# Decays and queries of a chunked decay attention read straight out of PSUM, one pair of score banks, a weight split moved to GpSimd

## The reference

```
for t in range(S):
    cur = einsum('bhd,bhe->bhde', u * k[t], v[t])
    y[t] = einsum('bhd,bhde->bhe', r[t], state + cur)
    state = w[t] * state + einsum('bhd,bhe->bhde', k[t], v[t])
x = moe(y)                                # 4 experts, causal softmax, top 2
out = x + relu(norm(x) @ w_ch1) @ w_ch2
```

## Time and profile before

| | us |
|---|---|
| median of 3 runs | 906.62 |
| lowest, highest | 905.15, 911.12 |
| span of the profiled execution, first to last instruction | 907.4 |
| busy in it: TensorE, VectorE, ScalarE, GpSimd | 843.7, 489.2, 362.3, 145.4 |
| mean granted clock of TensorE | 0.941 of full |

### The profile page before, as it was taken

One profiled execution on the slowest core, in us unless ns is written; L12 is line 12 of the kernel. 1 busy time (PEld: TensorE's weight loads), 2 busy tenths in 40 slices (PEclk: granted clock), 3 DMA queues, 4 the chain that ended last, 5 costly groups with the idle time before them and its releaser, 6 DMA issues.

```text
span 907.4 us, 16347 instructions
## 1 busy us (share of the span) xinstructions
PE 843.7 (93%) x5962; PEld 787.3 (87%) x5962; DVE 489.2 (54%) x1022; ACT 362.3 (40%) x714; POOL 145.4 (16%) x127
## 2 busy tenths in 40 slices
PE   3878877777999999999999999999999999999998
PEld 3777776677889889999988999998899999889998
DVE  4899999999753565222356522225562232556221
ACT  4666665756413454112344411234441123444111
POOL 4464656555400000000000000000000000000000
PEclk8587979978669999999999999999999999999999
DMA  5544645544330000000100000010000000000000
GB/s 152 149 96 104 162 104 108 171 116 91 71 122 1 1 1 1 18 18 22 52 1 1 1 18 18 20 54 1 1 1 19 18 10 10 1 1 2 18 18 18
DMA packets 94007, 40.69 MB, mean 45 GB/s; under 512 B 73712, under 2 KB 93296, under 8 KB 93936
## 3 DMA queue, kind: packets, MB, share of 16 engines
q1 hardware_dynamic: 93664, 38.55, 16.5%
q0 software_dynamic: 272, 1.18, 0.4%
HBM read 30.19 MB, written 9.54 MB: 44 GB/s over the span
## 4 chain that ended last, share of the span: by engine, by line
PE 75%; DVE 19%; issue 4%; ACT 1%; DMA 1%; DVEq 0%; POOL 0%; SPq 0%; ACTq 0%; POOLq 0%
PE sc_ps L1302 26%; PE tp L1420 17%; PE mx_ps L1342 8%; DVE grow L899 4%; DVE state L937 4%; PE tp L1330 4%; PE sc_ps L1437 3%; DVE suf L883 3%; PE tp L1302 3%; PE mx_ps L1302 3%; PE mx_ps L1437 2%; PE sc_ps L1319 2%; PE y_ps L1263 2%; DVE w_lo L957 1%; DVE at L915 1%
## 5 line engine op out<-in xcount | busy, mean ns | idle before, releaser
L858 ACT ACTIVATE hT_hi<-sc_ps 128x256 fp32r<-128x256 f32 x144 | 55.4, 385 | 203.0 <-PE sc_ps L1302 203.0
L1302 PE MATMUL sc_ps<-aT_hi,w_hi 128*128 128x256 f32 x432 | 123.5, 286 | 0.0
L1302 PE MATMUL sc_ps<-aT_hi,w_lo 128*128 128x256 f32 x432 | 122.3, 283 | 0.0
L1302 PE MATMUL sc_ps<-aT_lo,w_hi 128*128 128x256 f32 x432 | 122.2, 283 | 0.0
L1010 DVE TENSOR_REDUCE nmax<-sc_ps 128x1 f32<-128x768 f32 (+2 forms) x96 | 59.8, 623 | 87.6 <-PE sc_ps L1319 86.5
L684 POOL TENSOR_TENSOR rstd<-vare,power 128x1 f32<-128x1 f32 x24 | 13.2, 550 | 567.8 <-DVE vare L1058 567.8
L1181 DVE SCALAR_TENSOR_TENSOR hT_lo<-sc_ps,hT_hi 128x256 fp32r<-128x256 f32 x144 | 60.7, 424 | 72.8 <-ACT hT_hi L858 72.2
L1420 PE MATMUL tp<-w_hi,hT_hi 128*128 128x384 f32 x288 | 97.3, 338 | 0.0
L1420 PE MATMUL tp<-w_hi,hT_lo 128*128 128x384 f32 x288 | 96.8, 336 | 0.0
L1420 PE MATMUL tp<-w_lo,hT_hi 128*128 128x384 f32 x288 | 96.7, 336 | 0.0
L1263 PE MATMUL y_ps<-vc,at 128*128 128x64 f32 x384 | 71.5, 323 | 14.7 <-DVE state L928 8.9
(11 more groups left out here) (170 smaller groups left out, 1799.6 us busy)
## 6 DMA issues: line engine op xcount, KB each, us to landing
nat_w<-in_w SPq DMA_DIRECT2D x16, 288.0 KB, 3.3
nat_k<-in_k SPq DMA_DIRECT2D x16, 288.0 KB, 3.6
nat_r<-in_r SPq DMA_DIRECT2D x16, 288.0 KB, 3.9
vc<-in_v SPq DMA_DIRECT2D x32, 144.0 KB, 2.8
stage<-in_moe_w_ch SPq DMA_DIRECT2D x6, 768.0 KB, 5.6
x_scratch<-ystage SPq DMA_DIRECT2D x16, 288.0 KB, 3.0
out<-ost SPq DMA_DIRECT2D x24, 192.0 KB, 1.9
xs<-x_scratch SPq DMA_DIRECT2D x3, 1152.0 KB, 5.9
```

What stands on the lines that cost most here:

```text
L858: nc.scalar.activation(hT_hi[:, n % FT, :], sc_ps[:, n % 4 // 2, n % 2, 0:TF], ACT.Relu).then_inc(h_hi, 1)
L1302: last = pe.matmul(o, a, c, start=(i == 0), stop=(i == len(ops) - 1), skip_group_check=True)
```

## The change

- w is loaded with two neighbouring positions per partition and three blocks of 256 positions (runs of 384 bytes in DRAM in place of 1152), and its six transpositions write into a PSUM tile of its own, `w_ps`, with a step of two columns, so that w lies there in the order of time. The scans of `decays` and `growth` read w_ps; wT and its copy are gone. `decay_rows` transposes two units ahead, behind outputs(1) and ahead of key_values.
- r stays in PSUM in the order (c, p). `queries` moves from GpSimd to VectorE, multiplies it there by grow with a strided view of PSUM, and writes qhat; rT and its copy are gone. k is still copied by ScalarE, now with the stride on the side of the PSUM read.
- `a_ps` has one pair of banks instead of two, so `pairs` of one half waits for `masked` of the other.
- The low part of each w_ch2 piece is computed by GpSimd behind khat.
- `sums` moves behind `y_half` 1; semaphores are split accordingly.

```diff
-        wT = sb("wT", [P, S], on=p1)
-        rT = sb("rT", [P, S], on=p1)
+        w_ps = pb("w_ps", [P, 2 * 512], on=q1)
         tp1 = pb("tp1", [P, 2 * 512], on=q1)
-        a_ps = pb("a_ps", [P, G, 2, 512], on=q1)
+        a_ps = pb("a_ps", [P, 2, 512], on=q1)
...
+                sp.dma_start(nat_w[:, i % 2, :, :].rearrange("p h (j x) -> p h j x", j=PAIRS),
+                             of_unit(w, b, i).rearrange("b h (j p c) d -> p (b h) j (c d)", p=P, c=2)
+                             ).then_inc(rkw_in[i % 2], 16)
...
-            def queries(un, i):
-                pool.wait_ge(tp_out, prep_use(un, 2) + 1)
-                pool.wait_ge(grow_ok, un + 1)
-                pool.tensor_tensor(qhat[:, i % HP, :], rT[:, :], grow[:, :], ALU.mult).then_inc(qhat_ok, 1)
...
+            def low(piece, n):
+                staged, hi, lo, _ = piece
+                pool.wait_ge(stage_hi, n + 1)
+                pool.tensor_tensor(lo, staged, hi.bitcast(F32), ALU.subtract).then_inc(w2_split, 1)
...
-                    queries(un + 1, i + 1)
+                if not isinstance(un, int) and i >= 2:
+                    low(ffn_piece(b, 1, i - 2), b * (2 * CUTS) + (i - 2) * 2 + 1)
...
-                nc.scalar.activation(in_time((wT, kT, rT)[j][:, :]),
-                                     prep_bank(un, j).rearrange("x (c p) -> x c p", c=NR),
-                                     ACT.Copy).then_inc(tp_out, 1)
+                nc.scalar.activation(kT[:, :].rearrange("x (p c) -> x p c", c=NR),
+                                     tp1[:, 0:S].rearrange("x (c p) -> x p c", c=NR), ACT.Copy).then_inc(k_out, 1)
...
-                    done = dve.tensor_tensor_scan(backwards(suf, first, last - 1), backwards(wT, first + 1, last),
+                    done = dve.tensor_tensor_scan(backwards(suf, first, last - 1), backwards(w_ps, first + 1, last),
                                                   ones[:, 0:C - 1], 1.0, ALU.mult, ALU.mult)
...
-                    done = dve.tensor_tensor_scan(grow[:, first + 1:first + C], wT[:, first:first + C - 1],
+                    done = dve.tensor_tensor_scan(grow[:, first + 1:first + C], w_ps[:, first:first + C - 1],
                                                   ones[:, 0:C - 1], grow[:, first:first + 1], ALU.mult, ALU.mult)
...
+            def queries(un, i):
+                dve.wait_ge(r_full, un + 1)
+                dve.wait_ge(grow_ok, un + 1)
+                dve.tensor_tensor(qhat[:, i % HP, :].rearrange("x (p c) -> x p c", c=NR),
+                                  r_bank(un).rearrange("x (c p) -> x p c", c=NR),
+                                  grow[:, :].rearrange("x (p c) -> x p c", c=NR), ALU.mult).then_inc(qhat_ok, 1)
...
+            def decay_rows(un):
+                pe.wait_ge(pad_ok, un * PREP + 1)
+                if not isinstance(un, int) or un:
+                    pe.wait_ge(grow_ok, un)
+                for c in range(NR):
+                    first = c // 2 * (2 * P) + c % 2
+                    last = pe.transpose(w_ps[:, first:first + 2 * P - 1:2], channels(pad_w, c), ident[:, :])
+                last.then_inc(w_full, 1)
...
                 pe.wait_ge(khat_ok, un + 1)
-                pe.wait_ge(tp_out, khat_use(un))
+                pe.wait_ge(qhat_ok, un + 1)
...
-                if i >= 1:
-                    pe.wait_ge(at_ok, un * G + g - 1)
+                if i >= 1 or g:
+                    pe.wait_ge(at_ok, un * G + g)
```

More of the change, by code:

```diff
@@ L30, in build @@
     RUN = NR * D
+    PAIRS = S // (2 * P)
     PW = 2 * D
@@ L196, in build @@
         pad_ok = sem("pad_ok")
-        tp_full = sem("tp_full")
-        tp_out = sem("tp_out")
+        w_full = sem("w_full")
+        k_full = sem("k_full")
+        k_out = sem("k_out")
+        r_full = sem("r_full")
+        back_full = sem("back_full")
+        khn_ok = sem("khn_ok")
+        w2_split = sem("w2_split")
         suf_ok = sem("suf_ok")
@@ L314, in build, with r_bank @@
         PREP = 3
[L316 to L327, removed]
+        def r_bank(un):
+            if isinstance(un, int) and un == 0:
+                return a_ps[:, :, :].rearrange("p a n -> p (a n)")[:, 0:S]
             return tp1[:, 0:S]
@@ L972, in _ @@
             growth(0, 0)
-            dve.wait_ge(tp_out, prep_use(0, 1) + 1)
+            dve.wait_ge(k_out, 1)
             dve.tensor_tensor(khat[:, 0, :], kT[:, :], suf[:, :], ALU.mult).then_inc(khat_ok, 1)
-            dve.wait_ge(tp_out, prep_use(0, 2) + 1)
-            dve.wait_ge(grow_ok, 1)
-            dve.tensor_tensor(qhat[:, 0, :], rT[:, :], grow[:, :], ALU.mult).then_inc(qhat_ok, 1)
+            queries(0, 0)
             sums(0)
@@ L996, in turn @@
                     growth(un + 1, i + 1)
-                if exists(un + 1):
                     masked(un, i, 1)
-                    sums(un + 1)
+                    queries(un + 1, i + 1)
                 if i >= 1:
                     y_half(un - 1, i - 1, 1)
+                if exists(un + 1):
+                    sums(un + 1)
                 if not isinstance(un, int) and i >= 2:
-                    for n in range(2):
-                        low(ffn_piece(b, n, i - 2), b * (2 * CUTS) + (i - 2) * 2 + n)
+                    low(ffn_piece(b, 0, i - 2), b * (2 * CUTS) + (i - 2) * 2)
             def maxima(b, n):
@@ L1192, in _ @@
             y_half(NU - 1, HP - 1, 0)
-            low(expert_piece(0), IN_LOOP)
+            low(expert_piece(0), 2 * IN_LOOP)
             y_half(NU - 1, HP - 1, 1)
@@ L1196, in _ @@
             for n in (1, 2):
-                low(expert_piece(n), IN_LOOP + n)
+                low(expert_piece(n), 2 * IN_LOOP + n)
             sequences(dve, walk)
@@ new lines, in key_rows, with query_rows @@
+            def key_rows(un):
+                pe.wait_ge(pad_ok, un * PREP + 2)
+                if not isinstance(un, int) or un:
+                    pe.wait_ge(khn_ok, un)
+                for c in range(NR):
+                    last = pe.transpose(tp1[:, c * P:(c + 1) * P], channels(pad_k, c), ident[:, :])
+                last.then_inc(k_full, 1)
+            def query_rows(un):
+                pe.wait_ge(pad_ok, un * PREP + 3)
+                if not isinstance(un, int) or un:
+                    pe.wait_ge(k_out, un + 1)
+                for c in range(NR):
+                    last = pe.transpose(r_bank(un)[:, c * P:(c + 1) * P], channels(pad_r, c), ident[:, :])
+                last.then_inc(r_full, 1)
@@ L1232, in pairs @@
                         o = (c - g * GC) * C
-                        last = pe.matmul(a_ps[:, g, hh, o:o + C], khat[rows, i % 2, cs], qhat[rows, i % HP, cs],
+                        last = pe.matmul(a_ps[:, hh, o:o + C], khat[rows, i % 2, cs], qhat[rows, i % HP, cs],
                                          start=True, stop=True)
@@ L1267, in _ @@
             pe.wait_ge(const_ok, 4)
-            for j in range(PREP):
-                to_channels(0, j)
+            decay_rows(0)
+            key_rows(0)
+            query_rows(0)
+            decay_rows(1)
             def turn(un, b, i):
@@ L1288, in turn @@
                 if exists(un + 1):
-                    to_channels(un + 1, 1)
+                    key_rows(un + 1)
                 pairs(un, i, 1)
                 if exists(un + 1):
-                    to_channels(un + 1, 2)
+                    query_rows(un + 1)
                 if i >= 1:
                     outputs(un - 1, i - 1, 1)
+                if exists(un + 2):
+                    decay_rows(un + 2)
                 key_values(un, b, i)
```

89 lines of the change are left out of this document (42 added, 47 removed).

## The result

| | us |
|---|---|
| before, median of 4 runs beside it | 908.87 (905.15 to 912.07) |
| changed, median of 4 runs | 885.97 (885.20 to 887.25) |
| ratio | 0.9749, 95% interval 0.9718 to 0.978 |
| profiled execution: span before, after | 907.4, 883.7 |

A forecast was written before the change was run, and what follows sets the result against it. VectorE was taken to set the pace in the first stage. Turns -17.3, start -3.4 and TensorE's clock +5 sum to -15.7 us, from the median of 906.62 to 890.9, say 891; range 883 to 907.

The forecast's parts named there:

- The turn: First-stage loop on VectorE: 13.66 us with weight pieces instead of 15.38, 13.29 without; 13 turns 176.1 against 193.4, saving 17.3.
- A scan out of PSUM: I take 0: VectorE scans reading PSUM instead of SBUF: no added time taken, with up to 0.06 us a scan allowed.
- queries 0.85: The queries operation, new on VectorE with a strided PSUM read: 0.85 us, taken from masked.
- The clock term, +5: TensorE at half clock finishes key_values late: about 2.2 us of wait in two to three of 13 turns, +5 us.
- The start, -3.4: Before the turns: savings from dropped copies and shorter growth groups, less queries, load and first unit's squares, net -3.4 us.
- The 0.5 for the load: At the start: loading w in runs of 384 bytes instead of 1152 costs 0.5 us; 0 in the loop.
- The 2.2 for the first unit's squares: At the start: about 2.2 us until the first unit's squares, which now end last before decays(1).
- The tail and the second stage: After turn 14: the tail and the second stage keep their order, with no term in the sum.
- Half-rate read: Rival: the strided PSUM read makes queries take 1.65 us, +11 us in all, giving 902; chance 0.15.
- Scans that pay for PSUM: Rival: each scan out of PSUM costs 0.06 us more, 10 us in all, giving 901; chance 0.10.
- The lock stays: Rival: growth scans still contend with GpSimd and stay near 3.7 us, about 20 us return, giving 911; chance 0.05.
- TensorE takes over: Rival: low clock at every turn's end, 29 us of waiting for key_values, giving 915, slower than before; chance 0.10.

The follow-up runs named there:

- e1: Changed kernel with the second low part moved back from GpSimd to VectorE, behind the first: 895.73 us, ratio 0.9849 to the kernel before.
- e3: Two changed kernels with queries altered: no step, query reordering left out, 881.64 us; PSUM read in sequence, 24-byte steps in SBUF, 892.76 us.
- e6: Changed kernel with key_values put ahead of decay_rows on TensorE: 885.01 us, ratio 0.9732 to the kernel before.
- e2: Changed kernel with ScalarE copying w_ps to SBUF again and all scans reading that copy: 912.22 us, ratio 1.0058 to the kernel before.
- e0: The changed kernel itself, unaltered, run as base for variants on the same chip: 884.68 us, ratio 0.9716 to the kernel before.
- e9: The changed kernel once more, unaltered, as base for variants on another chip: 884.53 us, ratio 0.9743 to the kernel before.
- e4: Changed kernel with GpSimd making khat ahead of the two ruk products: 861.85 us, ratio 0.9522; on a second chip 863.47 us, ratio 0.9512.
- e7: Changed kernel with both edits, e4's khat ahead of ruk and e1's second low part back on VectorE: 873.80 us, ratio 0.9621.

## Why the prediction came out as it did

**The turn was right, step by step.** From y_half(1): vdiag T+0.59 to T+1.77 (said: 0.58 to 1.75), next behind the low part T+2.24 (2.22), chain T+3.11 (3.09), second ruk product ends T+5.05 (5.06), masked(0) T+6.01 (6.02), to the first growth scan 3.58 (3.68), growth 2.26 (2.26), masked(1) 0.85, queries 0.87 (0.85). An undisturbed turn with pieces is 13.57 (13.66), one without 13.11 (13.29). Nine and four of these are 174.6, a saving of 18.8 where the prediction had 17.3. The 13 turns took 176.47, because 1.9 us of waits and small delays are in them; that this is so near the 176.1 of the prediction, which held no waits, is luck. That the low part would be given back in part by the chain is shown by e1. The place of sums, the single pair of score banks and the load of w in shorter runs were not tried alone.

**"A scan out of PSUM: I take 0"** and **"queries 0.85"** held: 398 ns in either memory, 951 beside 946. By the fixed parts in the Trainium skill (VectorE: DVE Perf Modes, "The TRN2 errata"), 58 and 120 cycles at 0.96 GHz, each scan would be 65 ns longer, as an estimate from that page; the decay scans show none of it, and this measurement decides. e3 shows why the second held: only the step in SBUF costs.

**The clock term, +5, was the step that failed.** The waits it counted are there: three turns of 13 wait for kv_ps, 3.8 us in all, where two to three turns of 2.2 were charged. It is also one of the prediction's own signs of being wrong ("if VectorE idles on kv_ps"). But each made its turn only 0.4 us longer, 1.2 in all, and e6, which removes them, is no faster. The prediction let the state chain wait for ruk when it priced the low part, and forgot the same cover when it priced a wait ahead of the chain. Without that term the sum is -20.7.

**The start, -3.4, was 6.1.** The 0.5 for the load was not there (nat_w lands in 3.4 us, 3.3 before, and the first scan gains 2.06 where -1.1 was reckoned). The 2.2 for the first unit's squares was an idle of 0.25 before the second unit's scans; 1.90 of wait for ruk stood ahead of sums instead. And the chain of turn 1 lost 2.2 of its 4.22, for which 1.40 was paid in the wait ahead of it.

**The tail and the second stage, taken as unchanged**, gave -1.84 and +1.20. In the tail the granted clock is 0.64 where it was 0.50. That this is why it is shorter was not tested.

Together, in us saved: 18.8 for 17.3 in the undisturbed turns; 1.2 lost on kv_ps, and 0.7 in smaller delays, for the 5 charged; 6.1 for 3.4 at the start; 0.6 net from the tail and the second stage, for nothing. That is 23.7 between the spans.

**The rivals.** Half-rate read: fell by e3 (949 without, 951 with the step). Scans that pay for PSUM: fell. The lock stays: fell, and e2, measured at 912, is what it would have looked like (forecast 911; that includes the +5 and a start that were off, so the nearness is in part luck). TensorE takes over: fell in this kernel. What of its clock costs time at all is not settled: over the 13 turns the mean granted clock was 0.91 in e0 and 0.87 in e9, the same kernel, and the turns took 177.56 and 175.37, the shorter at the lower clock; in two executions of the e4 kernel it was 0.89 and 0.96 from 14 to 205 us, at spans of 865.8 and 861.8. Why e1 and e7 wait longer for y_ps than the kernels without the second low part on VectorE is open too.

## What to carry to other kernels

Where VectorE and GpSimd both have two SBUF inputs, look for the operation of VectorE whose input already lies in PSUM and drop the copy; then ask which of GpSimd's products still stands beside a two-SBUF chain, and move it beside the one that no longer minds (e4 gained nearly as much again, by the place of one line). Check with a run that puts the old state back, as e2 does: a copy that costs ScalarE 0.8 us cost the kernel 27.5, because of where its reader then read. When one term of a sum rests on a cover (the chain waits for ruk anyway), put every other wait ahead of that point under the same cover; and if one side of an operation must step, try the PSUM side: with the steps measured here (512 bytes in PSUM, 24 in SBUF) that was free.

## What was not expected of the hardware

A step of six fp32 columns (24 bytes) in SBUF takes VectorE from 950 to 1535 ns for 768 columns, about as ScalarE's 1550 beside 800 before; a step of 128 columns (512 bytes) in a PSUM read costs neither engine anything (951 beside 949 ns, 810 beside 811). TensorE's transpositions into w_ps, which write every second column, are no slower than those that write in sequence by what the traces show: 320 ns in the mean beside 291 to 302 in the changed kernel's first profile, but 306 beside 306 and 309 in e0's (14 to 205 us), which is the same kernel.
